# Rotating four heads with one product per operand, and angles kept in turns

## The chip, the cores and the metric

The kernel runs on one core of a Trainium2 chip. The metric is the device time of one execution in microseconds. The kernel before took 549.72 us, the median of 3 runs (549.70 to 549.84).

## What is computed

The program chains three blocks. The change is in the first, a recurrence over 768 steps with a decaying, rotating state for 2 batches of 8 heads with 48 channels:

```python
mag = np.sqrt(a_re * a_re + a_im * a_im)
scale = np.minimum(mag, 0.999) / (mag + 1e-06)
a_re_n, a_im_n = (a_re * scale, a_im * scale)
for t in range(S):
    new_re = ar * S_re - ai * S_im
    new_im = ar * S_im + ai * S_re
    S_re, S_im = (new_re + kv, new_im)          # kv: outer product of k[t] and v[t]
    y[:, :, t] = np.einsum('bhd,bhde->bhe', q[:, :, t], S_re)
```

Its output goes through a mixture of 8 experts (each token to the expert with the largest logit, 384 to 1024 to 384 channels) and then through a dense two-layer network (384 to 2048 to 384).

## The kernel before

**Idea.** The product of the complex factors up to a step is exp(L + i*Phi), where L is the running sum of the logarithms of the magnitudes and Phi that of the angles. So q is multiplied by exp(L), k by exp(-L), both are rotated by Phi (that is, each gets a cosine half and a sine half), and the recurrence becomes masked attention within 256 steps plus a state that is carried on.

**Tiling.** The 768 steps are six blocks of 128, in three frames of two blocks (j = 0, 1). A frame is worked in eight groups g, each of four heads of one batch of one block. The tiles have the 128 steps on the partitions: a block of both batches is 768 columns (`BW`), one batch of it 384 (`UW`), one group 192.

**What is done for each frame f.** ScalarE and VectorE make the logarithms `lr` and the angles `th`. TensorE adds them up over the steps with a triangular matrix (`running`, L950, with `upto` or `after`) into PSUM. ScalarE takes the exponentials (L440, L441). VectorE brings the angle sums into range (`reduce_angle`, L654 to L658, called by `phase`): first it multiplies by 1/2pi and adds a large constant that rounds to a whole number, then it subtracts this constant and multiplies by -2pi, then it adds the sum from PSUM. ScalarE makes the sine `sn`, the absolute value, and the cosine `ph` (`sin_cos`, L453 to L457). VectorE scales q and k (`scale`, L634, L635).

**What is done for each group.** VectorE rotates (`rotate`): four products of 128x192, q by cosine (L698) and by sine (L699), k by cosine and by sine, into `q_rot` and `k_rot`, which hold for each head 48 cosine columns, a gap up to column 64 (`SINE`), and 48 sine columns (112 in all, `DP`). TensorE transposes the rotated tiles (L986, L989); ScalarE copies q out of PSUM (L470), and k is copied by VectorE in frame 0 (L707) and by ScalarE from frame 1 on (L474); TensorE makes the scores (L998), VectorE masks them (`mask_scores`, L716), TensorE applies them and the state to v (L1017, L1020) and updates the state (L1030, L1031), VectorE adds the state (`state`, L724), ScalarE writes out y (L478).

**Between frames.** The state is carried to the next frame's origin. TensorE sums the logarithms and the angles between the two origins (`totals_of`, L957, L958); VectorE picks the diagonal (L671), reduces (L677) and brings the 16 angles per row into range with the same `reduce_angle` (`hop_phase`); ScalarE takes their sine and cosine (L461 to L465); VectorE makes two factors and shifts the state (L686, L687, L736 to L739).

**Order.** Each engine has its own queue, written out by hand in the order of `attend` (one for VectorE, one for TensorE, one list for ScalarE), with semaphores between. In step s of frame f TensorE transposes group s, scores group s-1 and applies group s-2, and in steps 3 to 9 the next frame's preparation is woven in: its logarithm totals in step 3, logarithm sums in step 4, angle sums in steps 5 and 6, with `phase` for j = 0 in VectorE's step 5 and for j = 1 in step 6, the angle totals and `hop_phase` in step 7, the next frame's rotations 0, 1 and 2 in steps 7, 8 and 9, and `squared_sum` (L628) at the end of step 8. Rotations 0 to 2 of frame 0 stand before `attend`. In the last frame nothing is prepared; the first token tiles are transposed for the router in the same steps.

At the start POOL fills the constant tiles (`ident`, `upto`, `after`, `ones` and others) and then releases the semaphore `consts`, on which ScalarE, VectorE and TensorE wait before anything else.

Of the kernel before, what the change touches and what calls it, by code (L numbers as in the profile page):

```python
# [29 lines left out]
P = 128  # L30
# [4 lines left out]
def fused_attention_moe_mlp(nc, q_in, k_in, v_in, ar_in, ai_in, gate_in, alpha_in, w_in, out, shapes):  # L35
# [39 lines left out]
    with ctx:  # L75
# [14 lines left out]
        after = sb("after", [P, P])  # L90
        alpha = sb("alpha", [P, FB2])
# [32 lines left out]
        totals = ab("totals", [DP, BW])  # L124
# [50 lines left out]
        consts, act_passed = sem("consts"), sem("act_passed")  # L175
# [153 lines left out]
        def _(pool):  # L329
# [7 lines left out]
            def select(ap, op, fill, base, pattern, cm):  # L337
# [10 lines left out]
            pool.memset(kt[:, :, :, D:SINE], 0.0)  # L348
            then(pool.memset(half_pi[:, :], math.pi / 2))
# [8 lines left out]
                      allow_small_or_imprecise_dtypes=True).then_inc(consts, 1)  # L358

# [22 lines left out]
        def _(act):  # L382
# [67 lines left out]
            def sin_cos(f, j):  # L450
                table(TRIG)
                act.wait_ge(phi_ready, 2 * f + (j + 1))
                A(two(sn, j), two(ph, j), ACT.Sin).then_inc(phi_abs, 1)  # L453
# [3 lines left out]
                A(two(ph, j), two(ph, j), ACT.Sin, scale=-1.0, bias=half_pi[:, 0:1]).then_inc(trig_ready, 1)  # L457

            def hop_sin_cos(f):
                act.wait_ge(hop_phi, f)  # L460
                A(hop[:, 3, :], hop[:, 2, :], ACT.Sin).then_inc(hop_abs, 1)  # L461
# [3 lines left out]
                A(hop[:, 2, :], hop[:, 2, :], ACT.Sin, scale=-1.0, bias=half_pi[0:DP, 0:1]).then_inc(hop_trig, 1)  # L465
# [139 lines left out]
        def _(dve):  # L605
# [46 lines left out]
            def reduce_angle(out_ap, source, steps, n, ready):  # L652

                TS(out_ap, source, 1.0 / TWO_PI, ROUND, ALU.mult, ALU.add).then_inc(steps, 1)  # L654
                dve.wait_ge(steps, n + 1)
                TS(out_ap, out_ap, ROUND, -TWO_PI, ALU.subtract, ALU.mult).then_inc(steps, 1)
                dve.wait_ge(steps, n + 2)
                TT(out_ap, out_ap, source, ALU.add).then_inc(ready, 1)  # L658

            def phase(f, j):  # L660
# [3 lines left out]
                reduce_angle(by_b(two(ph, j)), sums(f, j, 1), phi_steps, 4 * f + 2 * j, phi_ready)  # L664
# [14 lines left out]
            def hop_phase(f):  # L679
                dve.wait_ge(hop_sums, 2 * f)  # L680
                reduce_angle(hop[:, 2, :], hop[:, 1, :], hop_steps, 2 * f - 2, hop_phi)
# [7 lines left out]
            def rotate(f, g):  # L689
# [607 lines left out]
```

## Time and profile before

| | |
|---|---|
| median of 3 runs | 549.72 us |
| the profiled execution | 548.02 us |
| its span (first to last instruction) | 546.1 us |
| mean granted TensorE clock | 0.952 of full speed |
| busy: TensorE, VectorE, ScalarE, POOL | 467.5, 363.7, 272.3, 42.9 us |

The profiled execution took 1.9 us more than its span and 1.7 us less than the median. Attention, with its loads, takes the first 166 us or so of the span, the router and the scattering of rows to about 203 us, the experts and the dense network the rest. An engine's busy time counts each instruction from its start to its end; instructions of one engine can overlap, since the next starts before the one ahead has written its last results.

### The profile page before, as it was taken

The page shows a single profiled execution, that of the slowest core. Times are in us where ns is not written, and L with a number is a line of the kernel's source. Part 1 is how long each engine was busy: PE and PEld are TensorE (multiplying, and loading weights), DVE is VectorE, ACT ScalarE, POOL GpSimd, SP SyncE. Part 2 cuts the span into 40 slices and gives each one's busy share as a digit, 9 for nine tenths or more (in the row PEclk, how much of TensorE's full clock was granted, in tenths as well). Part 3 has the DMA queues.
Part 4 walks back from the last instruction along what each step waited for, and adds up shares of the span by engine and source line. Part 5 has one row for each costly group of instructions (what it writes and reads, how often), then busy time and mean ns, then how long its engine had stood idle before and what let it go on. Part 6 is the DMA issues. An engine that isn't in the chain of part 4 may idle for free.

```text
span 546.1 us, 10002 instructions
## 1 busy us (share of the span) xinstructions
PE 467.5 (86%) x3752; PEld 417.7 (76%) x3752; DVE 363.7 (67%) x624; ACT 272.3 (50%) x431; POOL 42.9 (8%) x48
## 2 busy tenths in 40 slices
PE   0538976999996029999999999999999999999995
PEld 0237755777885029999999998989998899889985
DVE  2688798678534317776777776778747787487751
ACT  5996758673446017666666664433334333334212
POOL 2000000000001890000000000000002000110002
PEclk9959999999998559999999999999999999999999
DMA  8970000000000469667666666233324333230001
GB/s 323 424 294 2 3 1 1 2 1 2 2 3 2 159 188 324 182 192 215 205 195 199 200 189 190 89 99 104 96 78 145 102 101 114 70 108 0 1 0 60
DMA packets 22178, 63.69 MB, mean 117 GB/s; under 512 B 2928, under 2 KB 4464, under 8 KB 22128
## 3 DMA queue, kind: packets, MB, share of 16 engines
q1 hardware_dynamic: 20592, 58.27, 32.6%
q0 software_dynamic: 1536, 4.74, 2.3%
q8 instruction: 32, 0.52, 0.4%
q14 instruction: 18, 0.15, 0.1%
HBM read 58.27 MB, written 4.74 MB: 115 GB/s over the span
## 4 chain that ended last, share of the span: by engine, by line
PE 74%; DVE 8%; DMA 5%; issue 5%; POOL 3%; ACT 2%; SPq 2%; DVEq 0%; POOLq 0%; ACTq 0%
PE banks L1152 15%; PE banks L1150 15%; PE banks L1151 15%; PE banks L1160 7%; DMA vv<-v_rows 4%; PE banks L1161 3%; PE banks L998 3%; POOL rows_by_slot L369 3%; PE banks L986 2%; PE banks L1017 2%; PE banks L989 2%; PE banks L950 2%; PE banks L1020 1%; PE banks L1144 1%; PE banks L1046 1%
## 5 line engine op out<-in xcount | busy, mean ns | idle before, releaser
L870 DVE TENSOR_TENSOR w_lo<-raw_early,w_hi 128x768 fp32r<-128x768 f32 x84 | 80.0, 956 | 31.1 <-ACT w_hi L543 30.0
L588 ACT ACTIVATE g_hi<-g_all 128x512 fp32r<-128x512 f32 x48 | 30.3, 632 | 118.4 <-DVE g_all L923 118.4
L543 ACT ACTIVATE w_hi<-raw_early 128x768 fp32r<-128x768 f32 x84 | 70.4, 843 | 33.2 <-PE banks L1161 32.7
L1150 PE MATMUL banks<-w_hi,g_hi 128*128 128x384 f32 x192 | 65.1, 339 | 0.5 <-DVE g_lo L925 0.5
L1152 PE MATMUL banks<-w_hi,g_lo 128*128 128x384 f32 x192 | 65.0, 339 | 0.0
L1151 PE MATMUL banks<-w_lo,g_hi 128*128 128x384 f32 x192 | 64.9, 338 | 0.0
L1160 PE MATMUL banks<-h_hi_lo,w_hi 128*128 128x448 f32 x192 | 64.0, 378 | 0.9 <-DVE h_hi_lo L886 0.9
L925 DVE TENSOR_TENSOR g_lo<-g_all,g_hi 128x512 fp32r<-128x512 f32 x48 | 33.3, 693 | 44.2 <-ACT g_hi L588 44.2
L1150 PE MATMUL banks<-ys_hi,w_hi 128*128 128x512 f32 x144 | 56.1, 390 | 1.2 <-DVE ys_lo L900 1.2
L1152 PE MATMUL banks<-ys_hi,w_lo 128*128 128x512 f32 x144 | 57.1, 397 | 0.0
L1151 PE MATMUL banks<-ys_lo,w_hi 128*128 128x512 f32 x144 | 56.8, 394 | 0.0
L1150 PE MATMUL banks<-xs_hi,w_hi 128*128 x192 | 52.7, 274 | 0.1
L1151 PE MATMUL banks<-xs_lo,w_hi 128*128 x192 | 52.6, 274 | 0.0
L1152 PE MATMUL banks<-xs_hi,w_lo 128*128 x192 | 52.6, 274 | 0.0
L1161 PE MATMUL banks<-h_hi_lo,w_lo 128*128 128x224 f32 x192 | 50.9, 265 | 0.0
L921 DVE TENSOR_SCALAR g_neg<-banks,alpha 128x512 f32<-128x512 f32 x48 | 35.8, 746 | 7.5 <-PE banks L1152 7.4
L1160 PEld LDWEIGHTS banks<-h_hi_lo,w_hi 128*128 128x128 f32 x192 | 36.2, 189 | 4.4 <-DVE h_hi_lo L886 2.1
L1150 PEld LDWEIGHTS banks<-w_hi,g_hi 128*128 128x128 f32 x192 | 36.1, 188 | 3.4 <-DVE g_lo L925 1.5
L1151 PEld LDWEIGHTS banks<-w_lo,g_hi 128*128 128x128 f32 x192 | 36.1, 188 | 2.1
L1150 PEld LDWEIGHTS banks<-xs_hi,w_hi 128*128 128x128 f32 x192 | 36.7, 191 | 1.1 <-issue 0.4
L377 POOL DMA_INDIRECT out_rows<-xq,tok_slot x12 | 11.9, 991 | 324.5 <-ACT xq L597 322.7
L1152 PEld LDWEIGHTS banks<-xs_hi,w_lo 128*128 128x128 f32 x192 | 36.9, 192 | 0.0
(166 smaller groups left out, 981.2 us busy)
## 6 DMA issues: line engine op xcount, KB each, us to landing
raw_early<-weights SPq DMA_DIRECT2D x84, 384.0 KB, 3.5
raw_late<-weights SPq DMA_DIRECT2D x28, 384.0 KB, 3.5
xq<-q_rows SPq DMA_DIRECT2D x3, 776.0 KB, 16.6
xq<-rows_by_slot SPq DMA_DIRECT2D x12, 194.0 KB, 4.5
kk<-k_rows SPq DMA_DIRECT2D x3, 768.0 KB, 18.0
vv<-v_rows SPq DMA_DIRECT2D x3, 768.0 KB, 19.4
aa<-a_re_rows SPq DMA_DIRECT2D x2, 768.0 KB, 10.5
th<-a_im_rows SPq DMA_DIRECT2D x2, 768.0 KB, 11.9
```

Of the source, the lines that this page charges most:

```text
L369: pool.indirect_dma_start(xs_dram, bass.IndirectOffsetOnAxis(ap=slots_i[:, t:t + 1], axis=0), xq[:, x:x + XW], None).then_inc(scattered, 16)
L543: A(wh[:, slot, :], raw[slot], ACT.Copy).then_inc(w_hi, 1)
L588: A(gh[:, c % GBUF, :], gg[:, c % GBUF, :], ACT.Copy).then_inc(g_hi, 1)
L870: TT(wl[:, slot, :], raw[slot], wh[:, slot, :].bitcast(F32), ALU.subtract).then_inc(w_lo, 1)
L921: TS(gn[:, :], HM[c % HBUF][:, :], 0.0, alpha[:, i:i + 1], ALU.min, ALU.mult).then_inc(g_neg, 1)
L925: TT(gl[:, c % GBUF, :], gg[:, c % GBUF, :], gh[:, c % GBUF, :].bitcast(F32), ALU.subtract).then_inc(g_lo, 1)
L998: x = MM(SC[g % 2][:, c], lhsT=kT[:, g % 2, c], rhs=qT[:, g % 4, c], start=True, stop=True)
L1150: MM(o, lhsT=whi, rhs=mhi, start=first, stop=False)
L1151: MM(o, lhsT=whi, rhs=mlo, start=False, stop=False)
L1152: return MM(o, lhsT=wlo, rhs=mhi, start=False, stop=last)
L1160: MM(both, lhsT=whi, rhs=hs[:, slot, :, 0:n], start=first, stop=False)
L1161: return MM(o[:, 0:n], lhsT=wlo, rhs=hh[:, slot, 0:n], start=False, stop=last)
```

## The change

- `rotate` makes the cosine and the sine half of one operand in a single product. The cosines and sines now lie in one tile `cos_sin` (cosines in the first half, sines in the second); q or k is read twice through a broadcast dimension, and the output tile has 128 columns for each head instead of 112, so that it can be seen as 2 halves of 64. So a group has two products of 128x384 instead of four of 128x192.
- The angles are summed in turns: the triangular matrices and the ones for the angles hold 1/2pi instead of 1 (`upto_per_turn`, `after_per_turn`, `ones_per_turn`, made by POOL with three more memsets ahead of `consts` and two more selects behind it; TensorE waits once for them, on `turn_consts`, ahead of the first angle sums).
- `reduce_angle` has two instructions instead of three: round by adding and subtracting the large constant, then subtract from the sum.
- ScalarE's sines take 2pi as their factor.
- The transposes read columns 0 to 112 of the wider tiles. `totals` is laid over a tile that is used later.

```diff
@@ constant tiles, on POOL
             pool.memset(kt[:, :, :, D:SINE], 0.0)
+            pool.memset(ones_t[:, :], 1.0 / TWO_PI)
+            pool.memset(upto_t[:, :], 1.0 / TWO_PI)
+            pool.memset(after_t[:, :], 0.0)
             then(pool.memset(half_pi[:, :], math.pi / 2))
...
                       allow_small_or_imprecise_dtypes=True).then_inc(consts, 1)
+            select(upto_t[:, :], ALU.is_ge, 0.0, 0, [[1, P]], -1)
+            select(after_t[:, :], ALU.is_ge, -1.0 / TWO_PI, 0, [[1, P]], -1).then_inc(turn_consts, 1)
@@ tiles
-        ph = ab("ph", [P, 2 * BW])
-        sn = ab("sn", [P, 2 * BW])
-        qt = ab("q_rot", [P, 4, G4, DP])
-        kt = ab("k_rot", [P, 4, G4, DP])
+        cs = ab("cos_sin", [P, 2, 2 * BW])
+        ph, sn = cs[:, 0, :], cs[:, 1, :]
+        qt = ab("q_rot", [P, 4, G4, 2 * SINE])
+        kt = ab("k_rot", [P, 4, G4, 2 * SINE])
...
-        totals = ab("totals", [DP, BW])
+        totals = xT[0:DP, :, :].rearrange("p a c -> p (a c)")
@@ sines, on ScalarE (the same two factors in hop_sin_cos)
-                A(two(sn, j), two(ph, j), ACT.Sin).then_inc(phi_abs, 1)
+                A(two(sn, j), two(ph, j), ACT.Sin, scale=TWO_PI).then_inc(phi_abs, 1)
...
-                A(two(ph, j), two(ph, j), ACT.Sin, scale=-1.0, bias=half_pi[:, 0:1]).then_inc(trig_ready, 1)
+                A(two(ph, j), two(ph, j), ACT.Sin, scale=-TWO_PI, bias=half_pi[:, 0:1]).then_inc(trig_ready, 1)
@@ bringing angles into range, on VectorE
             def reduce_angle(out_ap, source, steps, n, ready):
-                TS(out_ap, source, 1.0 / TWO_PI, ROUND, ALU.mult, ALU.add).then_inc(steps, 1)
+                TS(out_ap, source, ROUND, ROUND, ALU.add, ALU.subtract).then_inc(steps, 1)
                 dve.wait_ge(steps, n + 1)
-                TS(out_ap, out_ap, ROUND, -TWO_PI, ALU.subtract, ALU.mult).then_inc(steps, 1)
-                dve.wait_ge(steps, n + 2)
-                TT(out_ap, out_ap, source, ALU.add).then_inc(ready, 1)
+                TT(out_ap, source, out_ap, ALU.subtract).then_inc(ready, 1)
@@ rotate, on VectorE
-                c, sine = (heads(two(t, j, b))[:, h:h + G4, :] for t in (ph, sn))
+                at = j * BW + b * UW + h * D
+                trig = cs[:, :, at:at + G4 * D].rearrange("p c (h d) -> p c h d", d=D)
                 for dst, src in ((qt, rows(f, j, b)), (kt, half(kk, f, j, b))):
-                    TT(dst[:, g % 4, :, 0:D], heads(src)[:, h:h + G4, :], c, ALU.mult)
-                    x = TT(dst[:, g % 4, :, SINE:DP], heads(src)[:, h:h + G4, :], sine, ALU.mult)
+                    x = TT(dst[:, g % 4, :, :].rearrange("p h (c d) -> p c h d", c=2)[:, :, :, 0:D],
+                           heads(src)[:, None, h:h + G4, :].to_broadcast([P, 2, G4, D]), trig, ALU.mult)
                 x.then_inc(rot_ready, 1)
@@ TensorE's queue
             for j in range(2):
                 L_sums(0, j)
+            pe.wait_ge(turn_consts, 1)
             for j in range(2):
                 Th_sums(0, j)
```

`Th_sums` and the angle `totals_of` take the new matrices, `L_sums` and the logarithm `totals_of` the old ones.

## Rows read from the trace of the kernel before

**Rows 1.** Busy time by stretch: from:to, length, busy us (count), PEclk, DMA share
```profile
27.00:41.00 14.00, 5.15 (x24) 4.80 (x24) 11.90 (x24) 13.78 (x14) 0.00 (x0) 0.57 0.76 298
...
60.00:85.00 25.00, 21.86 (x313) 17.16 (x311) 24.04 (x48) 16.29 (x26) 0.00 (x0) 1.00 0.00 1
...
136.00:172.00 36.00, 34.28 (x605) 30.47 (x603) 13.76 (x35) 15.47 (x30) 2.05 (x2) 1.00 0.01 3
```

**Rows 2.** VectorE's groups to 220 us: busy total, mean ns; idle before, releaser
```profile
L698 DVE TENSOR_TENSOR q_rot<-xq,ph 128x192 f32<-128x192 f32 x24 | 8.4, 351 | 3.5 <-PE banks L1031 3.5
...
L724 DVE TENSOR_TENSOR w<-banks,w 112x384 f32<-112x384 f32 x10 | 5.5, 552 | 4.9 <-PE banks L1031 4.9
...
L671 DVE TENSOR_TENSOR totals<-banks,own_row 112x768 f32<-112x768 f32 x4 | 3.8, 952 | 4.9 <-PE banks L958 4.9
```

**Rows 3.** VectorE, one ScalarE row, in order of time: start us, us, instruction
```profile
24.74 0.95 DVE L654 TENSOR_SCALAR ph<-banks 128x768 f32<-128x768 f32 x1
25.73 0.56 DVE L656 TENSOR_SCALAR ph<-ph 128x768 f32<-128x768 f32 x1
26.32 0.95 DVE L658 TENSOR_TENSOR ph<-ph,banks 128x768 f32<-128x768 f32 x1
27.19 0.95 DVE L634 TENSOR_TENSOR xq<-xq,aa 128x768 f32<-128x768 f32 x1
...
30.58 0.94 ACT L457 ACTIVATE ph<-ph,half_pi 128x768 f32<-128x768 f32 x1
...
33.93 0.35 DVE L699 TENSOR_TENSOR k_rot<-kk,sn 128x192 f32<-128x192 f32 x1
```

**Rows 4.** POOL, VectorE, ScalarE in order of time, first 11 us
```profile
1.09 0.20 POOL L343 MEMSET after<- 128x128 f32 x1
1.24 0.18 POOL L344 MEMSET turn<- 112x112 f32 x1
...
8.87 0.96 DVE L623 TENSOR_TENSOR t<-t,lr 128x768 f32<-128x768 f32 x1
...
10.02 0.83 ACT L416 ACTIVATE lr<-t 128x768 f32<-128x768 f32 x1
```

**Rows 5.** VectorE at 66 us, rotation between two other operations
```profile
66.06 0.55 DVE L724 TENSOR_TENSOR w<-banks,w 112x384 f32<-112x384 f32 x1
66.52 0.35 DVE L698 TENSOR_TENSOR q_rot<-xq,ph 128x192 f32<-128x192 f32 x1
...
67.59 0.68 DVE L716 TENSOR_TENSOR scores<-banks,upto 128x512 f32<-128x512 f32 x1
```

**Rows 6.** TensorE at 50 us, in order of time
```profile
50.16 0.90 PE L957 MATMUL banks<-lr,ones 128*112 128x384 f32 x2 [1.39 <-DVE lr L650]
```

**Rows 7.** TensorE's and VectorE's rows at 65 us
```profile
64.81 0.60 PE L989 MATMUL banks<-ident,k_rot 128*112 128x128 f32 x4
...
65.45 0.69 DVE L707 COPY kT<-banks 112x512 f32<-112x512 f32 x1
```

**Rows 8.** What TensorE and ScalarE waited for at frame change, 72 to 85 us
```profile
72.52 0.90 PE L957 MATMUL banks<-th,ones 128*112 128x384 f32 x2 [1.48 <-DVE ph L658]
...
78.98 0.22 ACT L461 ACTIVATE hop<-hop 112x16 f32<-112x16 f32 x1 [3.80 <-DVE hop L658]
...
84.61 1.48 ACT L416 ACTIVATE lr<-t 128x1536 f32<-128x1536 f32 x1 [2.17 <-DVE t L628]
```

**Rows 9.** TensorE at the second frame change, 122 to 131 us
```profile
122.12 0.90 PE L957 MATMUL banks<-th,ones 128*112 128x384 f32 x2 [0.87 <-DVE ph L658]
...
130.25 0.32 PE L1017 MATMUL banks<-vv,scores 128*64 128x48 f32 x4 [0.87 <-issue]
```

**Rows 10.** VectorE in the last frame, one rotation of it
```profile
151.12 0.36 DVE L698 TENSOR_TENSOR q_rot<-xq,ph 128x192 f32<-128x192 f32 x1 [1.78 <-PE banks L1031]
```

**Rows 11.** ScalarE's groups: Ln without and with a factor
```profile
L416 ACT ACTIVATE lr<-t 128x768 f32<-128x768 f32 x2 | 1.7, 826 | 0.0
...
L428 ACT ACTIVATE t<-t 128x768 f32<-128x768 f32 x2 | 1.6, 828 | 0.0
```

More of the change, by code:

```diff
@@ L90, in fused_attention_moe_mlp @@
         after = sb("after", [P, P])
+        ones_t = sb("ones_per_turn", [P, P])
+        upto_t = sb("upto_per_turn", [P, P])
+        after_t = sb("after_per_turn", [P, P])
         alpha = sb("alpha", [P, FB2])
@@ L174, in fused_attention_moe_mlp @@
         own_ready = sem("own_ready")
-        consts, act_passed = sem("consts"), sem("act_passed")
+        consts, turn_consts, act_passed = sem("consts"), sem("turn_consts"), sem("act_passed")
         im_squared, re_squared, u_ready = sem("im_squared"), sem("re_squared"), sem("u_ready")
@@ L456, in sin_cos @@
                 act.wait_ge(phi_abs, 4 * f + (2 * j + 2))
-                A(two(ph, j), two(ph, j), ACT.Sin, scale=-1.0, bias=half_pi[:, 0:1]).then_inc(trig_ready, 1)
+                A(two(ph, j), two(ph, j), ACT.Sin, scale=-TWO_PI, bias=half_pi[:, 0:1]).then_inc(trig_ready, 1)
             def hop_sin_cos(f):
                 act.wait_ge(hop_phi, f)
-                A(hop[:, 3, :], hop[:, 2, :], ACT.Sin).then_inc(hop_abs, 1)
+                A(hop[:, 3, :], hop[:, 2, :], ACT.Sin, scale=TWO_PI).then_inc(hop_abs, 1)
                 act.wait_ge(hop_abs, 2 * f - 1)
@@ L464, in hop_sin_cos @@
                 act.wait_ge(hop_abs, 2 * f)
-                A(hop[:, 2, :], hop[:, 2, :], ACT.Sin, scale=-1.0, bias=half_pi[0:DP, 0:1]).then_inc(hop_trig, 1)
+                A(hop[:, 2, :], hop[:, 2, :], ACT.Sin, scale=-TWO_PI, bias=half_pi[0:DP, 0:1]).then_inc(hop_trig, 1)
             def q_evacuate(f, g):
@@ L663, in phase @@
                 dve.wait_ge(Th_ready, 2 * f + (j + 1))
-                reduce_angle(by_b(two(ph, j)), sums(f, j, 1), phi_steps, 4 * f + 2 * j, phi_ready)
+                reduce_angle(by_b(two(ph, j)), sums(f, j, 1), phi_steps, 2 * f + j, phi_ready)
             def own_totals(i, f):
@@ L680, in hop_phase @@
                 dve.wait_ge(hop_sums, 2 * f)
-                reduce_angle(hop[:, 2, :], hop[:, 1, :], hop_steps, 2 * f - 2, hop_phi)
+                reduce_angle(hop[:, 2, :], hop[:, 1, :], hop_steps, f - 1, hop_phi)
             def hop_factors(f):
@@ L945, in _, with running, totals_of @@
             pe.wait_ge(consts, 1)
-            def running(f, j, t, to):
+            def running(f, j, t, to, through, beyond):
                 for b in range(B):
-                    x = MM(to[:, b, :], lhsT=(upto if j else after)[:, :], rhs=half(t, f, j, b), start=True, stop=True)
+                    x = MM(to[:, b, :], lhsT=(through if j else beyond)[:, :], rhs=half(t, f, j, b), start=True, stop=True)
                 return x
-            def totals_of(t, f, free, count):
+            def totals_of(t, f, unit, free, count):
                 pe.wait_ge(free, count)
                 for b in range(B):
-                    MM(CUM[0:DP, b, 0:UW], lhsT=ones[:, 0:DP], rhs=half(t, f - 1, 1, b), start=True, stop=False)
-                    x = MM(CUM[0:DP, b, 0:UW], lhsT=ones[:, 0:DP], rhs=half(t, f, 0, b), start=False, stop=True)
+                    MM(CUM[0:DP, b, 0:UW], lhsT=unit[:, 0:DP], rhs=half(t, f - 1, 1, b), start=True, stop=False)
+                    x = MM(CUM[0:DP, b, 0:UW], lhsT=unit[:, 0:DP], rhs=half(t, f, 0, b), start=False, stop=True)
                 x.then_inc(totals_made, 1)
@@ L970, in L_sums @@
                         pe.wait_ge(exp_ready, 2 * f + 1)
-                running(f, j, lr, sums(f, j, 0)).then_inc(L_ready, 1)
+                running(f, j, lr, sums(f, j, 0), upto, after).then_inc(L_ready, 1)
             def Th_sums(f, j):
@@ L979, in Th_sums @@
                         pe.wait_ge(phi_ready, 2 * f + 1)
-                running(f, j, th, sums(f, j, 1)).then_inc(Th_ready, 1)
+                running(f, j, th, sums(f, j, 1), upto_t, after_t).then_inc(Th_ready, 1)
             def transpose_group(f, g):
@@ L985, in transpose_group @@
                 for i in range(G4):
[L986 removed]
+                    pe.transpose(TRQ[0:DP, i * P:(i + 1) * P], qt[:, g % 4, i, 0:DP], ident[:, :])
                 pe.wait_ge(k_out, K_FREE + 8 * f + g)
                 for i in range(G4):
[L989 removed]
+                    x = pe.transpose(TRK[0:DP, i * P:(i + 1) * P], kt[:, g % 4, i, 0:DP], ident[:, :])
                 x.then_inc(transposed, 1)
```

6 lines of the change are left out of this document (2 added, 4 removed).

## The prediction

> **What bounds the kernel now.** I first read the chain of work that ended last, in order of time, then the busy time by stretch, then each engine's instructions in order of time through attention. All that the change touches lies ahead of about 166 us; behind it the router, the experts and the dense network run the same instructions in the same order, so whatever attention gives or takes is passed on whole. Within attention the limit changes. From 27 to 41 us ScalarE and VectorE are nearly full. From 60 to 85 us VectorE is busy 24.04 of 25 us. From 136 to 172 us it is busy 13.76 of 36 us and TensorE 34.28 [rows 1]. So a shorter VectorE instruction is worth its length only in the first stretches and at the frame changes. In the last frame a rotation waits 1.78 us until TensorE has freed its buffer, as other rotations there do [rows 10], and a faster rotation only waits longer. Frame 1 up to the next angle sums is led by ScalarE (logarithms, exponentials) and TensorE in the same way.
>
> **The price of a rotation.** The tempting sum takes the durations: four products of 351 ns against two of about 552 (the row of a 384-column product), 0.30 us a group and 7.2 us over 24 groups [rows 2]. That is wrong by more than half, since instructions overlap. At 66 us a rotation starts at 66.52 and the mask behind it at 67.59: four products take 1.07 us of the queue, 0.27 each. A 384-column operation (L724) starts at 66.06 and hands over at 66.52: 0.46 to 0.48 us [rows 5]. Two of these are 0.95, so a rotation gives 0.12 us. The ready signal moves by about as much: 3 x 0.27 + 0.35 = 1.16 before, 0.48 + 0.55 = 1.03 after.
>
> The trace of before has no product with a broadcast middle dimension and a gapped output over 2 x 4 x 48 elements. From below: the plain 384-column row. From above: 952 ns, the 768-column row, as if each element took double; this row has three free dimensions and a broadcast operand itself, and takes no more than plain 768-column rows (0.95 for L634) [rows 2, 3]. So I take 0.55 us, start to start 0.48.
>
> The Trainium skill says otherwise of the overlap ("VectorE: DVE Perf Modes", section "The DRAIN you can't avoid"): the next operation doesn't start until the pipeline is empty. Read as a start at the end of the one ahead, this contradicts the 0.27 us between starts of 0.35 us long products. By that rule a rotation would give 0.30 us. The measurement decides here; the rule stands as a rival below.
>
> **The price of an angle reduction.** L654 starts at 24.74, L656 at 25.73, L658 at 26.32, the next operation at 27.19: 0.99 + 0.59 + 0.87 [rows 3]. The middle step goes. The first still reads PSUM and does two operations with constants, the last still reads PSUM and one tile, so both keep their prices: 0.59 us less, six times. In `hop_phase` three steps of 16 columns become two: about 0.20 us less, twice; I bound this by 0 and 0.25. Together VectorE's queue loses 24 x 0.12 + 6 x 0.59 + 2 x 0.20 = 6.8 us.
>
> **ScalarE, TensorE, POOL.** A factor on an activation is free: Ln without takes 826 ns, with a factor (and a bias) 828 [rows 11]; the same number of activations and tables stays. I bound it by 0 and, for the case that Sin differs, 0.09 us each. TensorE has the same matmuls with other constants: nothing. Its added wait on `turn_consts` has the transposes and all else of TensorE queued behind it, but POOL releases it some 6 us into the run and the sums stand at 23 us: nothing. The three memsets, however, stand ahead of `consts`: at 0.14 us from start to start they delay every engine's start by 0.42 us [rows 4]. Most of it vanishes in the wait for the first loads. VectorE's second sum (L623 at 8.87) would start near 9.2 and end near 10.2, where ScalarE now begins L416 at 10.02 [rows 4]; from there ScalarE is busy without a gap to 23 us. So 0.18 us of delay reaches the rest; bounds 0 and 0.42. If the loads came earlier, it would be the whole 0.42. The shared place of `totals` adds no wait, since its two users are a whole step apart; the wider tiles change no count of columns.
>
> **Following the shift along the chain.** I give how much earlier each point comes.
> 1. *Start.* From 24.74 us VectorE runs both reductions, both scalings and rotation 0 without a gap, and TensorE begins to transpose when that rotation ends, at 33.93 + 0.35 = 34.28 [rows 3]. Two reductions and a rotation: 2 x 0.59 + 0.12 - 0.18 = 1.12 us. The cosines for it stand ready at 30.58 + 0.94 = 31.52 us [rows 3], or 31.70 with the late start, and it would begin at 32.1, so ScalarE doesn't take over; the slack is 0.4 us.
> 2. *To 50 us.* One more rotation stands ahead of L650, which releases TensorE's totals after 1.39 us of waiting [rows 6]: 1.24.
> 3. *To 63 us* TensorE's sums and ScalarE's exponentials alternate: still 1.24. The reduction at 63 us gains nothing: the copy behind it starts at 65.45, but TensorE's transposes end at 64.81 + 0.60 = 65.41, so the two are level today, and the 0.59 us turns into a wait for TensorE [rows 7].
> 4. *First frame change.* Rotation 7 (0.12), the second reduction (0.59), rotation 0 of the next frame (0.12) and the hop (0.20) stand on VectorE's own queue; TensorE waits 1.48 us for the reduction, ScalarE 3.80 for the hop: 2.27 at 79 us. One rotation more stands ahead of L628, for which ScalarE waits 2.17 us: 2.39 at 84.6 us [rows 8].
> 5. *Frame 1 to 113 us*: ScalarE and TensorE lead, 2.39.
> 6. *Second frame change.* No copy by VectorE stands behind the first reduction, so it counts: 0.59. Then rotation 7, the second reduction, a rotation and the hop as before, 0.12 + 0.59 + 0.12 + 0.20: 2.39 + 1.62 = 4.01. TensorE waits 0.87 us for the second reduction, so of the 1.3 us that come ahead of it some turn into TensorE's own work there; but the hop stands on VectorE's queue and passes the full shift to ScalarE's sines and copies, for the last of which (y) TensorE stands at 130.25 [rows 9].
> 7. *Last frame*: TensorE leads, nothing is added [rows 1, 10].
>
> Sum: 4.0 us. The profiled execution goes from 548.02 to 544.0. The median of the runs was 1.70 us above that execution; I keep this distance: 549.72 - 4.0 = **545.7 us**.
>
> **The rivals.**
> *A, the gain is eaten before the end.* TensorE and ScalarE stand close behind VectorE at both frame changes, and TensorE's clock (0.57 from 27 to 41 us [rows 1]) rises only near 42 us. If it rises at the same moment though work begins 1.1 us earlier, half of this is lost, 0.55. If one second reduction and one hop are covered as well, 0.8 each, some 1.8 to 2.4 us stay: about 547.6. For it: the levels in step 3 show how thin the slack is. Against it: the waits of 1.48, 3.80 and 2.17 us [rows 8]. Chance 0.19.
> *B, each instruction holds VectorE for its whole duration*, so that a rotation gives 0.30 us. Seven rotations stand in the chain above: 7 x 0.18 = 1.3 us more, 544.4. A case beside it with the same sign is that what I take as covered counts too, the whole 6.8 us of the queue: 542.9. The skill's section on the DRAIN leads here. Against it: rows 5. Chance 0.09.
> *C, slower: the new product costs two steps per element.* The place is L699's successor; start to start 0.87 instead of 0.48 (0.95 us long, the upper bound). A rotation then costs 1.74 - 1.07 = 0.67 us more, seven of them on the chain 4.7 us, against 4.01 - 7 x 0.12 = 3.2 us from the rest: 1.5 us slower, 551.2. It turns to slower where a product takes over 0.76 us of the queue, and is measurably slower from 0.84. For it: no row has this pattern. Against it: L671 [rows 2]. Chance 0.08.
> *D, no change:* the first-load slack is thinner than I read, and only the reductions at the start come through: within 1.1 us of before. Chance 0.10.
> My forecast, 544.5 to 546.8, has 0.54.
>
> **How the numbers follow.** A measurement of this kernel can tell 0.2%, 1.1 us. Faster by more: my forecast 0.54, B 0.09, A 0.19, together 0.82; within: 0.10; slower: 0.08. The range takes in A and the upper part of B: 543.8 to 548.2, and leaves out C, most of D and the far end of B.
>
> **What would show it.** In the trace of the changed kernel: 48 products of 128x384 near 0.55 us with 0.48 between starts; two steps of 0.99 and 0.87 in each reduction; the first transpose near 33.2 us; a new wait of VectorE for TensorE of about 0.6 us ahead of the copy that is now at 65.45; ScalarE's L416 of the next frame near 82.2; all behind attention 4 us earlier. The prediction is wrong if the product is longer than 0.6 us, if the clock rises late, or if a third engine takes over at a frame change.

## The result, and the profile after

The changed kernel took 544.3 us, the median of 4 runs (544.04 to 545.21), against 549.71 (549.42 to 549.84): a ratio of 0.9915 with a 95% interval of 0.990 to 0.9931, that is 3.8 to 5.5 us less (the quotient of the two medians is 0.9902, at the edge of this interval). A second series gave 544.89 (6 runs) against 549.33 (17 runs), ratio 0.9921 (0.9907 to 0.9935). The forecast was 545.7 us, 4.0 us less. By the median alone, 544.3 us, rival B (544.4 us) would have been as good as the forecast; what tells them apart are the stretches between events, below.

The profiled execution of the changed kernel took 545.21 us with a span of 543.4, only 2.8 us less than that of before (548.02), and was the slowest of its four. So the two traces that everybody would lay side by side differ by half of what the medians differ. The readings below therefore compare stretches between two events, not the ends.

The new forms, by groups of VectorE instructions up to 220 us (busy total, mean ns, idle before and its releaser):

```profile
L705 DVE TENSOR_TENSOR k_rot<-kk,cos_sin 128x384 f32<-128x384 f32 x24 | 13.2, 550 | 0.0
L705 DVE TENSOR_TENSOR q_rot<-xq,cos_sin 128x384 f32<-128x384 f32 x24 | 13.2, 550 | 3.8 <-PE banks L1038 3.8
...
L664 DVE TENSOR_TENSOR cos_sin<-banks,cos_sin 128x768 f32<-128x768 f32 x6 | 5.7, 957 | 0.2
L662 DVE TENSOR_SCALAR cos_sin<-banks 128x768 f32<-128x768 f32 x6 | 5.7, 953 | 2.6 <-PE banks L957 2.6
```

The product with the broadcast operand and the gapped output takes 550 ns, as the plain 384-column row of before [rows 2]. There are 48 instead of 96, and six reductions have two steps. VectorE at 65 us, in order of time (start us, us):

```profile
65.17 0.69 DVE L714 COPY kT<-banks 112x512 f32<-112x512 f32 x1 [0.52 <-PE banks L996]
65.78 0.55 DVE L731 TENSOR_TENSOR w<-banks,w 112x384 f32<-112x384 f32 x1
66.24 0.55 DVE L705 TENSOR_TENSOR q_rot<-xq,cos_sin 128x384 f32<-128x384 f32 x1
66.70 0.55 DVE L705 TENSOR_TENSOR k_rot<-kk,cos_sin 128x384 f32<-128x384 f32 x1
67.17 0.68 DVE L723 TENSOR_TENSOR scores<-banks,upto 128x512 f32<-128x512 f32 x1
```

From the start of the rotation to the mask it is 67.17 - 66.24 = 0.93 us, where [rows 5] had 1.07. The copy of k that started with no wait in [rows 7] now waits 0.52 us for TensorE's transposes (L996): the reduction ahead of it became shorter and the engine stands still for as long.

The start of the run:

```profile
23.27 1.76 DVE L636 TENSOR_TENSOR t<-t,lr 128x1536 f32<-128x1536 f32 x1 [3.47 <-ACT t L419]
26.19 0.96 DVE L662 TENSOR_SCALAR cos_sin<-banks 128x768 f32<-128x768 f32 x1 [1.16 <-PE banks L957]
27.18 0.96 DVE L664 TENSOR_TENSOR cos_sin<-banks,cos_sin 128x768 f32<-128x768 f32 x1
28.06 0.95 DVE L642 TENSOR_TENSOR xq<-xq,aa 128x768 f32<-128x768 f32 x1
...
33.38 0.55 DVE L705 TENSOR_TENSOR q_rot<-xq,cos_sin 128x384 f32<-128x384 f32 x1
```

The reduction is 0.99 + 0.88 us as forecast, and from its start to the first rotation it is 33.38 - 26.19 = 7.19 us where it was 33.12 - 24.74 = 8.38 before; the rotation begins there with this row, 0.81 us ahead of its last one in [rows 3]:

```profile
33.12 0.35 DVE L698 TENSOR_TENSOR q_rot<-xq,ph 128x192 f32<-128x192 f32 x1
```

But the first reduction starts 1.45 us later than before, and 1.16 of this is a wait for TensorE that isn't in the trace of before.

The frame changes. ScalarE's rows that answer to [rows 8], and the same hop in the second change:

```profile
77.62 0.22 ACT L469 ACTIVATE hop<-hop 112x16 f32<-112x16 f32 x1 [3.45 <-DVE hop L664]
...
83.11 1.48 ACT L424 ACTIVATE lr<-t 128x1536 f32<-128x1536 f32 x1 [2.03 <-DVE t L636]
...
125.10 0.22 ACT L469 ACTIVATE hop<-hop 112x16 f32<-112x16 f32 x1 [2.36 <-DVE hop L664]
```

ScalarE waits for the hop for 3.45 instead of 3.80 us, for L636 2.03 instead of 2.17. ScalarE's logarithm of the next frame starts at 83.11, 1.5 us earlier than before (84.61) and not at the forecast 82.2: the late start of the first reduction is still in it. In the second change TensorE starts the angle totals as soon as its own scores are done, with no wait for the reduction, and later stands still for 0.75 instead of 0.87 us, which answers to [rows 9]; the program has a wait for y there, the trace names no releaser ("issue"):

```profile
118.89 1.06 PE L1005 MATMUL banks<-qT,kT 112*128 112x128 f32 x8
119.78 0.81 PE L964 MATMUL banks<-th,ones_per_turn 128*112 128x384 f32 x2
...
127.36 0.32 PE L1024 MATMUL banks<-vv,scores 128*64 128x48 f32 x4 [0.75 <-issue]
```

And by stretch, as [rows 1] (from:to, length, busy TensorE, weight load, VectorE, ScalarE, POOL; granted clock, DMA share):

```profile
27.00:41.00 14.00, 5.47 (x25) 4.67 (x24) 11.63 (x18) 13.74 (x14) 0.00 (x0) 0.67 0.76 296
60.00:85.00 25.00, 22.94 (x332) 18.29 (x331) 23.33 (x38) 17.51 (x26) 0.00 (x0) 1.00 0.01 1
136.00:172.00 36.00, 33.10 (x592) 29.62 (x588) 12.34 (x29) 16.51 (x32) 2.05 (x2) 0.95 0.01 3
```

VectorE is still nearly full from 60 to 85 us. In the last frame it is idle most of the time, as before.

**Where the time went.** The table gives, for each kernel, the time from one event to the next in its profiled execution, each event the start of an instruction (the first column is A itself, K-end goes to the end of the span, and a difference can be off by 0.02 us from rounding): A the first reduction's first step, B the first rotation, C and D the reductions of frame 1 (j = 0, 1), E ScalarE's first hop activation (the sine, L461 before), F the next ScalarE logarithm (L416 before), G and H the reductions of frame 2, I its first hop activation, J VectorE's copy of the logits, K the first expert matmul.

```
                           A     A-B    B-C    C-D   D-E   E-F    F-G    G-H   H-I    I-J    J-K   K-end
before                   24.74  8.38  29.86   6.95  9.05  5.63  28.59   6.33  8.47  43.56  37.26  337.28
changed                  26.19  7.19  29.32   6.81  8.11  5.49  28.77   5.71  7.51  43.46  36.75  338.09
changed, again           25.65  7.20  29.05   6.82  8.11  5.50  28.76   5.71  7.52  43.46  37.43  337.99
rotation_only            26.34  8.39  28.94   6.82  8.92  5.49  29.87   6.20  8.32  43.43  37.18  337.70
angles_only              25.47  7.19  29.20   6.95  8.26  5.63  30.02   5.74  7.66  43.56  36.87  337.05
fills_behind             25.32  7.18  29.80   6.82  8.11  5.50  29.77   5.71  7.52  43.46  37.04  337.87
long_first_of_frame1     24.99  7.19  29.79   6.82  8.12  5.49  29.70   5.70  7.52  43.46  36.91  337.81
long_seconds             25.32  7.20  28.92   6.81  8.71  5.49  28.58   5.70  8.12  43.43  37.66  337.66
early_old_rotation       25.43  7.19  29.19   6.96  8.25  5.63  28.52   5.74  7.66  43.56  37.15  337.32
last_frame_old_rotation  25.66  7.19  29.06   6.81  8.12  5.49  28.76   5.71  7.52  43.46  36.45  338.27
busy_short_first         25.51  7.19  29.33   6.82  8.12  5.49  28.77   5.71  7.52  43.45  37.75  337.94
busy_short_all           25.08  7.19  28.31   6.81  8.12  5.49  29.48   5.71  7.52  43.46  36.56  338.27
```

Seven columns repeat to 0.03 us between kernels that have the same instructions there: A-B, C-D, D-E, E-F, G-H, H-I, I-J. In these the change gives 1.19 + 0.14 + 0.94 + 0.14 + 0.62 + 0.96 + 0.10 = 4.09 us. The others (A, B-C, F-G, J-K, K-end) differ by 0.9 to 1.6 us between kernels with the same instructions in them; they hold the first loads or stretches in which TensorE has been idle and starts again. Between the two traces they took back 1.45 - 0.54 + 0.18 - 0.51 + 0.81 = 1.39 us, and 4.09 - 1.39 = 2.7 us is the difference of the spans. What moves B-C and F-G is in the main TensorE's clock (last section).

### The profile page after: what moved, and what is told of

The parts are those of the page before. It is cut to its first block, busy times and chain, and to the rows that moved or that the text cites. A ratio compares the mean times of both kernels' runs of the same rounds, so it can differ in the third digit from the quotient of the medians.

```text
span 543.4 us, 9953 instructions
## 1 busy us (share of the span) xinstructions
PE 468.0 (86%) x3752; PEld 417.9 (77%) x3752; DVE 356.9 (66%) x568; ACT 272.4 (50%) x431; POOL 43.9 (8%) x53
## 4 chain that ended last, share of the span: by engine, by line
PE 76%; DVE 6%; DMA 5%; issue 4%; POOL 3%; ACT 2%; SPq 2%; DVEq 0%; POOLq 0%; ACTq 0%
PE banks L1160 15%; PE banks L1158 15%; PE banks L1159 15%; PE banks L1168 7%; DMA vv<-v_rows 4%; PE banks L1169 4%; PE banks L1005 3%; POOL rows_by_slot L377 3%; PE banks L993 2%; PE banks L996 2%; PE banks L957 2%; PE banks L1024 2%; PE banks L1027 1%; PE banks L1053 1%; PE banks L1152 1%
## 5 line engine op out<-in xcount | busy, mean ns | idle before, releaser
L932 DVE TENSOR_TENSOR g_lo<-g_all,g_hi 128x512 fp32r<-128x512 f32 x48 | 33.2, 693 | 44.2 <-ACT g_hi L596 44.2
```

The source lines that it names most:

```text
L932: TT(gl[:, c % GBUF, :], gg[:, c % GBUF, :], gh[:, c % GBUF, :].bitcast(F32), ALU.subtract).then_inc(g_lo, 1)
```

## Experiments

Each edit is against the changed kernel unless it says otherwise. All were run in three groups, each beside the kernel before: 549.33 us (17 runs), 549.56 (17) and 549.58 (11). The changed kernel itself ran only ahead of them (4 runs) and in the first group (6 runs); where a kernel of the second or third group is compared with it, the middle of these ten runs, 544.6 us, or the 544.89 us of the six is meant.

### The changed kernel again

> The changed kernel once more, unaltered. Theory T1 (what differs between the two profiled executions at the start, TensorE still slow at 24 us so that the first angle sums end 1.5 us late, is an accident of one execution): in another execution the first reduction on VectorE begins at about 24.9 us without a wait, and the end comes about 1.1 us earlier than in the profiled execution of 545.21 us. Theory T2 (the later release of the constants always brings it): the wait of 1.2 us ahead of the first reduction is there again. Median by either: 544.3 +- 0.5 us, ratio to before 0.990 to 0.993.

544.89 us (6 runs, 544.32 to 545.78). VectorE's first reduction with its wait:

```profile
25.65 0.96 DVE L662 TENSOR_SCALAR cos_sin<-banks 128x768 f32<-128x768 f32 x1 [0.63 <-PE banks L957]
```

The wait is 0.63 us, not 1.16 and not 0: neither theory holds as written. What differs is TensorE. The rows are the second half of its logarithm sums and the first half of its angle sums, of before, of the changed kernel and of its repetition (start us, us; an x4 row is four passes, and a pass is one record of the trace):

```profile
21.57 1.72 PE L950 MATMUL banks<-lr,upto 128*128 128x384 f32 x4
23.12 1.45 PE L950 MATMUL banks<-th,after 128*128 128x384 f32 x4
```

```profile
21.77 2.77 PE L957 MATMUL banks<-lr,upto 128*128 128x384 f32 x4
24.33 1.82 PE L957 MATMUL banks<-th,after_per_turn 128*128 128x384 f32 x4
```

```profile
21.77 2.55 PE L957 MATMUL banks<-lr,upto 128*128 128x384 f32 x4
24.16 1.45 PE L957 MATMUL banks<-th,after_per_turn 128*128 128x384 f32 x4
```

The same four passes take 1.72, 2.77 and 2.55 us; four passes at the full rate take 1.45. The rate rises near 22, 25 and 24 us, and the first angle sums (the row behind) follow. The traces' clock entries agree: the first full-clock entry begins at 22.09, 25.07 and 23.98 us.

### The rotation alone

Against the kernel before: the tiles `cos_sin`, `q_rot` and `k_rot` and the loop of `rotate` as changed, nothing of the angles.

```diff
                 for dst, src in ((qt, rows(f, j, b)), (kt, half(kk, f, j, b))):
-                    TT(dst[:, g % 4, :, 0:D], heads(src)[:, h:h + G4, :], c, ALU.mult)
-                    x = TT(dst[:, g % 4, :, SINE:DP], heads(src)[:, h:h + G4, :], sine, ALU.mult)
+                    x = TT(dst[:, g % 4, :, :].rearrange("p h (c d) -> p c h d", c=2)[:, :, :, 0:D],
+                           heads(src)[:, None, h:h + G4, :].to_broadcast([P, 2, G4, D]), trig, ALU.mult)
```

> Only the rotation as two products of 128x384; angles in radians with three steps, no added fills. By the ledger of the prediction seven rotations stand on the chain with 0.12 us each: 0.8 us less than before. If durations counted (0.30 us a rotation): 2.1 us less. If all 24 counted at 0.12: 2.9 us less.

548.84 us (12 runs), 0.5 us under before where 0.8 was expected, ratio 0.9997 (0.9985 to 1.0009): not told from no change. The columns show the edit where it lies: C-D 6.95 to 6.82, D-E 9.05 to 8.92, E-F 5.63 to 5.49, G-H 6.33 to 6.20, H-I 8.47 to 8.32, I-J 43.56 to 43.43: 0.13 to 0.15 us for each rotation, six of them, 0.81 us, with two more in B-C that can't be told from its accidents. That excludes 0.30 us for a rotation. The interval of the ratio ends at 0.8 us less, so it holds the six and not eight. This kernel has none of the added fills, and yet the wait ahead of the first reduction is there, which refutes T2:

```profile
26.34 0.96 DVE L654 TENSOR_SCALAR cos_sin<-banks 128x768 f32<-128x768 f32 x1 [1.00 <-PE banks L951]
```

### The angles alone

```diff
-                    x = TT(dst[:, g % 4, :, :].rearrange("p h (c d) -> p c h d", c=2)[:, :, :, 0:D],
-                           heads(src)[:, None, h:h + G4, :].to_broadcast([P, 2, G4, D]), trig, ALU.mult)
+                    TT(dst[:, g % 4, :, 0:D], heads(src)[:, h:h + G4, :], c, ALU.mult)
+                    x = TT(dst[:, g % 4, :, SINE:DP], heads(src)[:, h:h + G4, :], sine, ALU.mult)
```

> Only the angles in turns with two steps; rotation in four products, into the wider tiles. By the ledger: five of six reductions at 0.59 and two hops at 0.20, less 0.18 for the fills: 3.2 us less than before. If the rotation were what carried the gain: under 1 us.

545.38 us (6 runs), ratio 0.9928 (0.9915 to 0.9941): 4.0 us less, interval 3.2 to 4.7, where 3.2 was expected. The columns: A-B 1.19, D-E 0.79, G-H 0.59, H-I 0.81, and nothing in C-D, 3.38 us in all, before the fills. So the angles carry the change, and the two parts add up (0.5 + 4.0 against 4.4 for both in the same group).

### The added fills behind the release

```diff
-            pool.memset(ones_t[:, :], 1.0 / TWO_PI)
-            pool.memset(upto_t[:, :], 1.0 / TWO_PI)
-            pool.memset(after_t[:, :], 0.0)
             then(pool.memset(half_pi[:, :], math.pi / 2))
...
                       allow_small_or_imprecise_dtypes=True).then_inc(consts, 1)
+            pool.memset(ones_t[:, :], 1.0 / TWO_PI)
+            pool.memset(upto_t[:, :], 1.0 / TWO_PI)
+            then(pool.memset(after_t[:, :], 0.0))
             select(upto_t[:, :], ALU.is_ge, 0.0, 0, [[1, P]], -1)
```

> The changed kernel with the three added fills moved behind the release of the constants. By the ledger the fills cost 0.18 us, so 0.2 us less than the changed kernel, ScalarE's and VectorE's rows to 23 us at the times of before. If T2 holds, the first reduction then begins without a wait and 1.2 us more come with it: 1.4 us less.

544.56 us (6 runs, 542.91 to 545.92), 0.3 us under the changed kernel with intervals of about +- 0.8 and +- 0.9 us: not told apart. The first reduction has no wait here, but angles_only, with the fills in front, has none either. The trace shows why it hangs on the execution. ScalarE's first square starts at 5.97 us here and at 6.41 in the changed kernel, 0.44 earlier as the three fills are; but the second square waits for its load:

```profile
8.37 0.84 ACT L413 ACTIVATE lr<-th 128x768 f32<-128x768 f32 x1 [1.55 <-DMA th<-a_im_rows]
```

```profile
7.85 0.84 ACT L413 ACTIVATE lr<-th 128x768 f32<-128x768 f32 x1 [0.60 <-DMA th<-a_im_rows]
```

This load landed at 7.6 to 8.6 us in the twelve traces, and sets where ScalarE's queue begins. With a load at 7.85 the fills cost 0.20 us (VectorE's L636 at 23.27 against 23.07); here, with a load at 8.37, the row is at 23.64 without them. The other traces say how far this goes: with and without the fills VectorE's row stands 15.26 or 15.27 us behind the second square wherever the load comes at 8.0 us or later, and with the fills it never comes before 23.26. So the fills cost 0.15 us at a load of 7.85 (0.05 of the 0.20 is the load's own), 0.35 at the earliest, 7.64, and nothing from 8.0 on.

### One reduction long, the first of frame 1

```diff
+                if long:
+                    TS(out_ap, source, ROUND, None, ALU.add).then_inc(steps, 1)
+                    dve.wait_ge(steps, n + 1)
+                    TS(out_ap, out_ap, ROUND, None, ALU.subtract).then_inc(steps, 1)
+                    dve.wait_ge(steps, n + 2)
+                else:
                     TS(out_ap, source, ROUND, ROUND, ALU.add, ALU.subtract).then_inc(steps, 1)
...
+                             long=(f == 1 and j == 0))
```

> The changed kernel with three steps instead of two in one reduction alone, that of frame 1, j = 0 (near 63 us). By the ledger this reduction gained nothing, since TensorE's transposes end level with it: the wait of 0.5 us ahead of the copy of k shrinks to nothing, the copy moves by at most 0.1 us against the reduction's start (2.5 us behind it instead of 2.47), and the median stays within 0.1 us of the changed kernel. If every reduction counted: 0.6 us more, and the copy 3.06 us behind the start.

545.17 us (5 runs, 543.84 to 545.28). From the reduction's start to the copy of k behind it:

```profile
61.97 0.96 DVE L666 TENSOR_SCALAR cos_sin<-banks 128x768 f32<-128x768 f32 x1 [0.38 <-PE banks L967]
...
64.45 0.69 DVE L724 COPY kT<-banks 112x512 f32<-112x512 f32 x1
```

64.45 - 61.97 = 2.48 us, against 65.17 - 62.70 = 2.47 in the changed kernel, and C-D is 6.82 in both. So the added step of 0.59 us is taken out of a wait and moves nothing behind it: in the trace this reduction gives nothing, as forecast. The median doesn't show it. It is 0.3 us above the 544.89 and 0.6 above the 544.6, not within 0.1, and 0.6 is what the rival expected; with an interval of about +- 0.8 us it holds both. The columns decide: where this trace differs from the changed kernel's, it is in A, B-C and F-G, and the edit is not in those.

### Two reductions long, the second of frames 1 and 2

The same edit with `long=(f >= 1 and j == 1)`.

> The changed kernel with three steps in the two reductions of frames 1 and 2 with j = 1 (near 70 and 119 us). By the ledger both stand on the chain: 1.2 us more than the changed kernel; from the start of the second reduction of frame 1 to ScalarE's first hop activation 8.7 us as before the change less 0.3 (that is 8.7 instead of 8.1). If they are covered: no change.

545.75 us (5 runs, 545.36 to 546.56), 1.1 us more than the middle of the changed kernel's ten runs (544.6). D-E is 8.71 instead of 8.11 and H-I 8.12 instead of 7.51, 0.60 and 0.61 us. These two stand on the chain whole (expected: 1.2 us, and D-E 8.7).

### The old rotation early, and the old rotation in the last frame

Four products instead of two under `if not (f == NF - 1 and g >= 3)`, and in the other kernel under `if f == NF - 1 and g >= 3`.

> The changed kernel with the rotation in four products everywhere except in the last frame from its fourth group on. By the ledger all that the rotation gives lies here, 7 x 0.13 us: 0.9 us more than the changed kernel, about what angles_only measured (545.4 us).

> The changed kernel with the rotation in four products in the last frame from its fourth group on. By the ledger these rotations wait for TensorE anyway: from ScalarE's second hop activation to the logits' copy 43.4 to 43.5 us as in the changed kernel, median within 0.1 us of it. If TensorE waited for rotations there: 5 x 0.13 = 0.6 us more.

544.88 (6 runs) and 544.50 us (5 runs) cannot be told apart; the early one is 0.3 us above the changed kernel's 544.6 where 0.9 was expected. The columns tell more: with the early rotations old, C-D, D-E, E-F, H-I and I-J are those of angles_only (6.96, 8.25, 5.63, 7.66, 43.56), 0.7 us with G-H's 0.03; with the last frame's old, every one of them is that of the changed kernel, I-J at 43.46. A rotation there has its wait ahead of it, the one of [rows 10]:

```profile
147.33 0.36 DVE L705 TENSOR_TENSOR q_rot<-xq,cos_sin 128x192 f32<-128x192 f32 x1 [1.78 <-PE banks L1044]
```

The 0.10 us of I-J belong to the rotation in it that comes before the last frame is led by TensorE.

### TensorE kept busy ahead of the sums

Matmuls whose result nobody reads, in TensorE's queue:

```diff
+            for _ in range(30):
+                MM(CUM[:, 0, 0:UW], lhsT=ident[0:DP, :], rhs=w0[:, 0:UW], start=True, stop=True)
             for j in range(2):
                 L_sums(0, j)
             pe.wait_ge(turn_consts, 1)
```

> The changed kernel with 30 matmuls of 128x384 ahead of the first sums on TensorE, whose result nobody reads. In the profiled executions so far TensorE's first angle sums end between 24.6 and 26.3 us, and VectorE waits for them in five of six. Theory C (TensorE works at half its rate for some us after a long idle time, and when the full rate comes differs from execution to execution): with TensorE busy from 5 us the sums run at the full rate at once, the first reduction begins at 24.9 to 25.0 us without a wait, and the end comes 0.7 to 1.2 us earlier than in the changed kernel. Rival D (the wait is for the angles or the loads): the same wait as before and no gain.

550.16 us (12 runs), 5.3 us above the changed kernel (544.89), where 0.7 to 1.2 less was expected. A mistake of size: each matmul is two passes (60 records for 30 matmuls), 0.65 us together at the full rate, so they ran to 26.5 us and the sums came late:

```profile
5.13 21.55 PE L1109 MATMUL banks<-w,ident 112*128 112x384 f32 x60 [5.13 <-POOL prior L363]
26.52 1.46 PE L957 MATMUL banks<-lr,after 128*128 128x384 f32 x4
...
29.11 1.45 PE L957 MATMUL banks<-th,after_per_turn 128*128 128x384 f32 x4
```

The sums themselves run at 1.45 us for four passes from the first. So a busy TensorE does bring them the full rate, but they start 7 us late, and the first reduction waits 5.58 us.

### TensorE kept busy in three gaps

The same with 30 matmuls, 16 more between the angle sums and the first transposes (on the same bank, after the exponentials have read it), and 66 on a free bank while the rows are scattered.

> As busy_before_sums, and TensorE also kept busy from 26 us to the first transposes (16 matmuls) and while the rows are scattered (66 matmuls). Theory C: the transposes and scores from 34 to 42 us run at twice their rate, which takes 2 to 3 us from that stretch (two thirds of it are TensorE's), and the 36 transposes at 200 us lose 1 to 1.5 us; all in all 4 to 5 us less than the changed kernel, near 540 us. If the rate doesn't matter there: 544.5 us.

567.82 us (5 runs, 566.95 to 568.41), 23 us above the changed kernel and 18 above before, for the same reason: the last 66 ran from 176.9 to 222.5 us, and the first expert matmul came 54.67 instead of 37 us behind J.

### The same with fewer

17 matmuls ahead of the sums:

> As busy_before_sums with 17 matmuls instead of 30. There each took 0.65 us at the full rate, two passes of 0.32, so that 30 of them ran to 26.5 us and held up the sums. 17 should end near 18 us. Theory C: the four sums then take 1.46 us each from 19.1 us on as they did there, the first reduction begins at about 24.9 us without a wait for them, and the median is 0.5 to 1 us under the changed kernel. Rival D: no change in the wait.

545.28 us (6 runs, 544.28 to 546.39). TensorE and VectorE:

```profile
5.13 14.00 PE L1109 MATMUL banks<-w,ident 112*128 112x384 f32 x34 [5.13 <-POOL prior L363]
19.55 1.56 PE L957 MATMUL banks<-lr,after 128*128 128x384 f32 x4 [0.41 <-DVE lr L658]
20.94 1.45 PE L957 MATMUL banks<-lr,upto 128*128 128x384 f32 x4
22.23 1.45 PE L957 MATMUL banks<-th,after_per_turn 128*128 128x384 f32 x4
```

```profile
25.51 0.95 DVE L662 TENSOR_SCALAR cos_sin<-banks 128x768 f32<-128x768 f32 x1
```

The sums take 1.56, 1.45 and 1.45 us and the reduction doesn't wait for them; the same holds in busy_short_all. The median doesn't show the 0.5 to 1 us that were expected: it is 0.4 us above 544.89. In the profiled execution the load was the latest of all (8.57 us), which puts the reduction at 25.51 by VectorE's own queue; for the other five runs the cause is not shown.

17, 9 and 38 matmuls in the three gaps:

> As busy_three_gaps with 17, 9 and 38 matmuls instead of 30, 16 and 66, so that they end before the work they stand ahead of. Theory C: four transposes from 33 to 42 us take 0.6 us instead of 1.07 and the scores 1.06 instead of 1.92 us, as they did there, 2 to 3 us less to 42 us; the rows' transposes at 200 us are all at the full rate; all in all 3.5 to 5 us less than the changed kernel, about 540.5 us. If the rate hardly lies on the chain: under 1 us less.

543.77 us (5 runs, 542.77 to 544.10), ratio 0.9891 to before (0.987 to 0.9912): 1.1 us under the changed kernel of the first group (544.89) and 0.8 under the middle of its ten runs, not 3.5 to 5; that is what the second half of the expectation names, the rate hardly on the chain. The rates came as expected:

```profile
26.38 7.76 PE L1117 MATMUL banks<-w,ident 112*128 112x384 f32 x18 [1.83 <-ACT t L449]
33.98 0.60 PE L993 MATMUL banks<-ident,q_rot 128*112 128x128 f32 x4
...
36.49 0.62 PE L993 MATMUL banks<-ident,q_rot 128*112 128x128 f32 x4 [1.47 <-DVE qT L718]
...
37.38 1.06 PE L1005 MATMUL banks<-qT,kT 112*128 112x128 f32 x8
```

Four transposes take 0.60 and the scores 1.06 us where the changed kernel has 1.07 and 1.92. The first scores are masked 38.79 - 32.27 = 6.5 us after the first rotation instead of 41.57 - 33.38 = 8.2, but at the end of B-C 28.31 against 28.92 to 29.80 is left. ScalarE's queue holds the next frame's logarithms and exponentials until then and copies q of group 2 only behind them, early transposes or not; it has no idle time in this trace from 9 to 51 us:

```profile
41.31 1.47 ACT L431 ACTIVATE aa<-aa 128x1536 f32<-128x1536 f32 x1
42.69 0.58 ACT L478 ACTIVATE qT<-banks 112x512 f32<-112x512 f32 x1
```

F-G is not helped (29.48), since its gap was left as it was and its stretch at half the clock is a long one here; J-K is 36.56, the row transposes at the full rate from the first, but they wait for their rows, and other executions came to 36.45 without. It is the fastest kernel of the study, by little.

## Why the prediction was right, point by point

**The price of a rotation**: 0.12 us forecast, 0.13 to 0.15 measured. The trace gives 0.47 us from start to start of products that are 0.55 long. The rule of the Trainium skill ("VectorE: DVE Perf Modes", "The DRAIN you can't avoid"), read as a start only when the pipeline is empty, would have given 0.30 us, and rotation_only excludes that. The same section adds that a next operation that isn't held starts earlier, which the prediction left out; the 0.27 and 0.47 us between starts agree with that. Rival B is refuted as far as it rests on the 0.30. Its other half, that all 6.8 us of the queue count, falls by the reduction at 63 us and by the last frame (long_first_of_frame1, last_frame_old_rotation). That the first median, 544.3 us, lies next to B's 544.4 and under the forecast's own 544.5 to 546.8 is chance; the second, 544.89, lies in it. **The product's own length**: 0.55 taken, 0.55 measured, so rival C falls.

**The price of a reduction**: 0.59 forecast, 0.59 measured in A-B (1.19 for two), G-H and, put back, in long_seconds (0.60, 0.61). The hop: 0.20 forecast; D-E gives 0.79 - 0.59 = 0.20 in angles_only, H-I 0.81 - 0.59 = 0.22. That refutes rival D, by which only the start would have come through.

**The steps of the ledger.** Step 3, that the reduction at 63 us gives nothing, is shown by angles_only (C-D 6.95 as before), by the wait of 0.52 us and by long_first_of_frame1. Step 4, forecast from D to F: two rotations, one reduction, one hop, 1.03 us; measured 0.94 + 0.14 = 1.08. Step 6, G to I: forecast 1.62, measured 0.62 + 0.96 = 1.58; a tenth is lost to a mask that now waits for its scores (it starts 0.57 us behind the last product, not 0.46, and G-H is 0.62, not the 0.59 + 0.13 of its parts). Step 7, nothing in the last frame: 0.10 was left there, an eighth rotation that I had counted as covered. Step 1's late start: 0.18 forecast, 0.20 in the two profiled executions, 0.15 of it by the fills; where the load lands at 8.0 us or later there is none.

Steps 1 and 2 hold two rotations that lie in B-C, 0.24 forecast, and they are the least sure, since TensorE's clock moves B-C too. Two pairs of traces have the clock alike there. In early_old_rotation and long_seconds (half the clock from 30.2 to 40.5 us and from 30.2 to 40.4) the work also begins at about the same time, and old and new rotation differ by 29.19 - 28.92 = 0.27 us, what two rotations give elsewhere. In the kernel before and long_first_of_frame1, which is the changed kernel up to C (28.9 to 42.6 us and 29.0 to 42.7), it is 29.86 - 29.79 = 0.07; there the first rotation begins 0.94 us earlier against the same clock, and some 0.2 us more go into the half rate, by my estimate from the two differences.

Together: 4.0 forecast; 4.09 in the repeating columns, plus 0.07 to 0.27, less 0 to 0.35 for the fills with a load between 8.57 and 7.64 us: 3.8 to 4.35.

**What was not foreseen.** The forecast took one profiled execution as if its rows were the kernel's. The execution of before was a lucky one: 1.5 us under the median of 45 later runs (549.5), with TensorE's full rate from 22 us on instead of 25 and no wait at the first reduction, which six of the nine later traces without added matmuls have (0.27 to 1.16 us). That of the changed kernel was the slowest of its four. The step "median minus ledger" survived this, because it kept the distance between execution and median out of the sum; the claim beside it, that the profiled execution would go to 544.0, missed by 1.2 us (545.21), and so did "first transpose near 33.2 us" (it is at 34.50), the logarithm near 82.2 (at 83.11) and "all behind attention 4 us earlier": VectorE's copy of the logits, J, is at 168.56 against 171.57, 3.0 us. Rival A had named TensorE's rate as a danger, at 42 us and with 0.55 us; the traces show it at four places, in both kernels, and with the clock alike some 0.2 us were lost to it up to C, not 0.55 (the pair of traces above). Its other half, a second reduction and a hop that are covered, is refuted by long_seconds.

**The median's difference**, 4.4 and 5.4 us in two series, lies above the ledger's 3.8 to 4.35, but both intervals (3.6 to 5.1, 3.8 to 5.5) hold 4.0 as well as 4.35. Whether the accidents fall a little better in the changed kernel isn't settled by these runs.

## What to carry to other kernels

Price an instruction that is removed by the time from start to start of its neighbours, not by its duration: here 0.12 us (measured 0.13) and 0.30 us for the same edit. Then walk the chain and ask at each place who else is ready at that moment; of about 7 us taken from VectorE's queue some 4 reached the end. And check the repeatability before two traces are compared by their ends: stretches between two events repeated to 0.03 us where the ends differed by 1 to 2.

## What the runs showed of the hardware

TensorE's passes of 128x384 take 0.64 us from start to start after the engine has been idle and 0.32 later. In the first sums the step came between 22 and 25 us for nearly the same start (18.9 to 19.5 us). The view of a stretch before it prints a granted clock of 1.00, which is no reading: the trace has no clock entry yet. Its first entry, full clock, begins with the step, at 22.09 us before, 25.07 in the changed kernel and 23.98 in its repetition. With matmuls from 5 us on (busy_short_first) it begins at 10.8 us, and the sums are at 0.32 us from the second pass on. Behind that the entries are at one of two levels, 0.50 and 1.00, that is 1.2 and 2.4 GHz, and the time of the rise differs from execution to execution. The changed kernel and angles_only at 94 us, after TensorE had stood idle for four us:

```profile
94.00:97.00 3.00, 3.00 (x27) 2.91 (x23) 2.57 (x3) 0.39 (x1) 0.00 (x0) 0.54 0.00 0
97.00:98.00 1.00, 1.00 (x22) 0.88 (x21) 0.35 (x1) 0.98 (x3) 0.00 (x0) 1.00 0.00 0
```

```profile
94.00:97.00 3.00, 3.00 (x28) 2.91 (x27) 2.29 (x5) 0.16 (x1) 0.00 (x0) 0.50 0.00 0
97.00:98.00 1.00, 1.00 (x7) 1.00 (x6) 0.00 (x0) 0.98 (x3) 0.00 (x0) 0.50 0.00 0
```

The one is at the full clock from 97 us on, the other not yet. By the entries the clock is at half from 93.3 to 96.8 us in the one and from 91.4 to 98.3 in the other, and their F-G differ by 30.02 - 28.77 = 1.25 us. All fourteen traces split this way: in the nine with the shorter stretch F-G is 28.5 to 28.8 us, in the five with the longer one (rotation_only, angles_only, fills_behind, long_first_of_frame1, busy_short_all) 29.5 to 30.0, whatever the edit. So the same instructions get the clock back at different moments, and in F-G that is about 1 us. B-C goes the same way in the ten traces without added matmuls: 29.8 to 29.9 us in the three with the longer stretch at half the clock (before, fills_behind, long_first_of_frame1; 28.9 to 42.6 us in the first), 28.9 to 29.3 in the seven with a shorter one (30.8 to 41.1 us in the repetition). Over whole runs the mean granted clock goes with the time only in part: of the changed kernel's ten runs the two at 0.947 are the slowest (545.70, 545.78), the four at 0.957 take 544.12 to 544.75, those at 0.953 544.04 to 545.21.

The Trainium skill ("TensorE: Matmul & The Clock Gate", "Part 1: The HAM clock gate") says that the moment isn't tied to the start of the kernel and so varies from run to run; the traces agree (22 to 25 us for the same start, and the two lengths at 94 us).
